# Windowed attention and two feed-forward layers: first chunk's tap products summed and transposed on TensorE, first unit in two halves, another order of softmax, loads and weight preparation

## The reference

```python
w = softmax(weight_gen)                      # over the 7 taps
out = np.einsum('bshk,bskhg->bshg', w, x_unf)  # x_unf: this token and the 6 before
h = x @ w_in1;  g = h * np.cos(h);  x = g @ w_out1
h = x @ w_in2;  g = np.maximum(0.01 * h, h); out = g @ w_out2
```

## Time and profile before

| what | us |
|---|---|
| median of 3 runs | 1177.1 (1176.54 to 1181.43) |
| the profiled execution | 1180.46 |
| its span | 1178.7 |
| PE busy | 1151.8 |
| DVE busy | 905.8 |
| ACT busy | 738.6 |
| POOL busy | 94.8 |

### The profile page before, as it was taken

One profiled execution on the slowest core, in us unless ns is written; L12 is line 12 of the kernel. 1 busy time (PEld: TensorE's weight loads), 2 busy tenths in 40 slices (PEclk: granted clock), 3 DMA queues, 4 the chain that ended last, 5 costly groups with the idle time before them and its releaser, 6 DMA issues.

```text
span 1178.7 us, 23306 instructions
## 1 busy us (share of the span) xinstructions
PE 1151.8 (98%) x10180; PEld 960.2 (81%) x10180; DVE 905.8 (77%) x857; ACT 738.6 (63%) x809; POOL 94.8 (8%) x87
## 2 busy tenths in 40 slices
PE   7879999999999999999999999999999999999998
PEld 5658888887878888888888888888888888888876
DVE  7778798787987869688686978868698786968533
ACT  5657675766847657575665756557575665757544
POOL 4764000000000000000000000000000000000000
PEclk9879999999999999999999999999999999999999
DMA  9400101001010010100001010010101001000000
GB/s 268 144 2 1 34 1 37 12 1 48 1 46 3 1 48 2 48 1 17 32 2 48 2 48 1 1 48 1 48 1 48 2 1 48 1 14 1 9 7 28
DMA packets 15277, 32.68 MB, mean 28 GB/s; under 512 B 5068, under 2 KB 9546, under 8 KB 14920
## 3 DMA queue, kind: packets, MB, share of 16 engines
q1 hardware_dynamic: 15176, 31.19, 8.4%
HBM read 24.89 MB, written 6.29 MB: 26 GB/s over the span
## 4 chain that ended last, share of the span: by engine, by line
PE 90%; DVE 4%; ACT 2%; POOL 2%; issue 1%; ACTq 0%; DVEq 0%; POOLq 0%
PE slot L940 41%; PE acc_a L940 27%; PE acc_b L940 18%; DVE g_lo L710 1%; PE slot L1136 1%; POOL prods L282 1%; DVE gate L774 1%; POOL prods L288 1%; PE acc_b L913 0%; DVE prods L282 0%; PE slot L885 0%; ACT gate L607 0%; ACT L656 0%; ACT whole L603 0%; PE slot L872 0%
## 5 line engine op out<-in xcount | busy, mean ns | idle before, releaser
L940 PE MATMUL acc_a<-g_hi,out_hi_lo 64*128 64x512 f32 x2000 | 698.9, 389 | 0.0
L710 DVE TENSOR_TENSOR g_lo<-gate,g_hi 128x1024 fp32r<-128x1024 f32 x256 | 319.7, 1249 | 115.8 <-ACT g_hi L548 115.2
L940 PEld LDWEIGHTS acc_a<-g_hi,out_hi_lo 64*128 64x128 f32 x2000 | 369.6, 185 | 36.0
L940 PE MATMUL acc_b<-g_hi,out_hi_lo 64*128 64x512 f32 x1000 | 389.8, 390 | 8.9 <-DVE g_lo L710 7.5
L940 PE MATMUL acc_a<-g_lo,out_hi_lo 64*128 64x512 f32 x1000 | 388.1, 388 | 0.0
L940 PE MATMUL acc_b<-g_lo,out_hi_lo 64*128 64x512 f32 x1000 | 387.8, 388 | 0.0
L548 ACT ACTIVATE g_hi<-gate 128x1024 fp32r<-128x1024 f32 x256 | 271.4, 1060 | 104.4 <-PE acc_b L940 82.9
L940 PE MATMUL slot<-x_a_hi,in_a_lo 64*128 64x512 f32 x1024 | 300.8, 395 | 1.6 <-DVE gate L788 1.3
L940 PE MATMUL slot<-x_a_hi,in_a_hi 64*128 64x512 f32 x1024 | 297.2, 388 | 0.0
L940 PE MATMUL slot<-x_a_lo,in_a_hi 64*128 64x512 f32 x1024 | 297.1, 388 | 0.0
L940 PE MATMUL slot<-x_b,in_b_hi 64*128 64x512 f32 x1024 | 296.9, 387 | 0.2 <-DVE x_b L724 0.2
(11 more groups left out here) (87 smaller groups left out, 1058.0 us busy)
## 6 DMA issues: line engine op xcount, KB each, us to landing
x_win<-in_x SPq DMA_DIRECT2D x14, 960.0 KB, 4.7
out<-result SPq DMA_DIRECT2D x16, 384.0 KB, 2.4
out_raw<-in_moe_w_out SPq DMA_DIRECT2D x2, 1024.0 KB, 14.1
taps_w<-in_weight_gen SPq DMA_DIRECT2D x2, 560.0 KB, 8.2
out_raw<-in_moe_w_out SPq DMA_DIRECT2D x2, 512.0 KB, 11.0
in_a_raw<-in_moe_w_in SPq DMA_DIRECT2D x1, 1024.0 KB, 9.0
in_b_raw<-in_moe_w_in SPq DMA_DIRECT2D x2, 512.0 KB, 10.8
in_a_raw<-in_moe_w_in SPq DMA_DIRECT2D x2, 384.0 KB, 6.3
```

The costliest lines, as they stand in the source:

```text
L710: nc.vector.tensor_tensor(g_lo[:, q % 2, :], gate[:, q % 2, :], g_hi[:, q % 2, :].bitcast(FP32), ALU.subtract)\
L940: return nc.tensor.matmul(to, w[rows, :], x[rows, :], start=start, stop=stop)
```

## The change

- **Chunk 0's attention.** DVE only multiplies. Each of the seven products is given to PE, which multiplies it with the identity and accumulates in the slot (`sum_tap`, 16 matmuls of fp32 data for each tap): sum and transposition in one. Four buffers `prods` rotate. `raise_clock` runs 4 products instead of 12, and no more of them between the steps.
- **Softmax.** The first part holds chunk 0 alone, the second chunks 1 and 2; the later parts stand at other steps.
- **First unit.** Its four elementwise stages and the split are done in halves of 512 columns.
- **ACT.** Its queue issues chunk 0's own window; both early Exp stand first; two pieces of columns instead of three stand ahead of `split_high`, and two quarters of `w_out1`'s high part behind it. The third piece follows within steps 0 and 1, with POOL doing its scaling.
- **Loads.** SP loads weights for chunks 0 to 2 first, the column pieces with half of `w_out1` between them, and chunk 1's window last of these.
- **POOL.** Another order, shown below; DVE's last additions of chunk 1 stand one step later (`ATT_END` 6), and the split of chunk 1's input behind the step's pending part.

```diff
-        ATT_DVE, ATT_POOL, ATT_END = 2, 9, 5
+        ATT_DVE, ATT_POOL, ATT_END = 2, 9, 6
-        SOFT_CHUNKS = [(0, 2), (2, 3), (3, 6), (6, 11), (11, C)]
+        SOFT_CHUNKS = [(0, 1), (1, 3), (3, 6), (6, 11), (11, C)]
-        SOFT_START, EXP_AT, SOFT_END = [[(1, 9), (2, 14), (3, 14)], [(1, 13), (2, 16), (3, 16)],
-                                        [(1, 15), (3, 9), (4, 9)]]
+        SOFT_START, EXP_AT, SOFT_END = [[(1, 8), (2, 13), (4, 13)], [(1, 10), (3, 10), (5, 10)],
+                                        [(1, 13), (3, 13), (5, 13)]]
...
-            for instruction in attention(0, dve):
-                instruction()
+            for n in range(taps):
+                if n == 1:
+                    softmax_subtract(1)
+                    dve.wait_ge(x_zeroed, 2 * batch)
+                    dve.wait_ge(halo_loaded[0], 64)
+                if n >= 4:
+                    dve.wait_ge(tap_summed, n - 3)
+                multiply_tap(dve, x_win, 0, taps - 1 - n, n % 4).then_inc(tap_ready, 1)
...
+            def sum_tap(slot, n):
+                tap = prods[:, n % 4, :]
+                def first_dims(j, start=False, stop=False):
+                    for k in range(2):
+                        rows = slice(k * DB, (k + 1) * DB)
+                        ins = nc.tensor.matmul(slot[:, k, j * DB:(j + 1) * DB],
+                                               tap[rows, j * dim:j * dim + DA], ident[rows, rows],
+                                               start=start, stop=stop)
+                    return ins
...
-            raise_clock(12)
-            for n in range(1, ATT_STEPS):
-                pe.wait_ge(att, n)
-                raise_clock(4)
-            pe.wait_ge(att, ATT_STEPS)
-            transpose_input(slots[INPUT_STEP % SLOTS])
+            raise_clock(4)
+            for n in range(taps):
+                pe.wait_ge(tap_ready, n + 1)
+                ins = sum_tap(slots[INPUT_STEP % SLOTS], n)
+                ins.then_inc(tap_summed if n < taps - 1 else filled, 1)
             keep_clock(WARM)
...
-            for n, cols in enumerate(HI_PIECES):
-                act.wait_ge(in_loaded[n], 48)
...
+            act.dma_start(x_win[:, halo:, :].rearrange("p t d -> p (t d)"), x_rows[:, 0:row])\
+                .then_inc(own_loaded[0], 16)
+            exponentials(0)
+            exponentials(1)
+            for n in range(2):
+                column_highs_a(n)
+                column_turns(n)
+                column_highs_b(n)
+            split_high(-1, INPUT_STEP, 0)
+            out_high(0)
+            out_high(1)
+            first_read(-1, STEPS - 1)
+            for step in range(STEPS):
+                step_of(0, step)
+                if step == 0:
+                    column_highs_a(2).then_inc(w1_a_read, 1)
+                if step == 1:
+                    column_highs_b(2)
```

More of the change, by code:

```diff
@@ L313, in attention @@
             yield rest_of_window
[L314 removed]
+            yield third
             yield lambda: tap(3, 3)
@@ L599, in first_read @@
                 slot = slots[step % SLOTS][:, :, :].rearrange("p a n -> p (a n)")
+                if unit(i, q) == 0:
+                    for cols, done in ((slice(0, N), unit_act), (slice(N, None), whole_ready)):
+                        nc.scalar.activation(whole[:, 0, cols], slot[:, cols], ACT.Identity, bias=0.25)\
+                            .then_inc(done, 1)
+                    return
                 if step in FIRST_UNITS:
@@ L624, in step_of @@
                     split_second_high(i, step)
-                if step == FIRST_INPUT_SPLIT and input_splits(i, step):
-                    split_high(i, FIRST_INPUT_STEP, i + 1)
                 if kind(i, step) == "output":
@@ L785, in step_of @@
                     leave_res_b(second_phase(i - 1))
-                if in_first:
+                if in_first and unit(i, q) == 0:
+                    for cols, ready, n, done in ((slice(0, N), unit_act, 2, unit_dve),
+                                                 (slice(N, None), cos_ready, 1, g_ready)):
+                        dve.wait_ge(ready, n)
+                        nc.vector.scalar_tensor_tensor(gate[:, 0, cols], slot[:, cols], RADIANS,
+                                                       gate[:, 0, cols], ALU.mult, ALU.mult)\
+                            .then_inc(done, 1)
+                elif in_first:
                     dve.wait_ge(cos_ready, first_units(i, q))
@@ L879, in transpose_input, with last_dims @@
                 ins.then_inc(filled, 1)
+            def sum_tap(slot, n):
[7 more added lines that the diff above has]
+                    return ins
+                def last_dims(j):
+                    for k in range(2):
+                        rows = slice(k * DB, (k + 1) * DB)
+                        nc.tensor.matmul(slot[0:DB, k, N // 2 + j * DB:N // 2 + (j + 1) * DB],
+                                         tap[rows, j * dim + DA:(j + 1) * dim], ident[rows, rows],
+                                         start=False, stop=False)
+                first_dims(0, start=n == 0)
+                for j in range(J):
+                    last_dims(j)
+                for j in range(1, J):
+                    ins = first_dims(j, stop=n == taps - 1 and j == J - 1)
+                return ins
             def transpose_output(slot):
```

248 lines of the change are left out of this document (172 added, 76 removed).

## The result

The changed kernel is slower by 0.6%: 1185.5 us (median of 4 runs, 1184.57 to 1186.81) against 1177.3 for the kernel before (4 runs, 1176.54 to 1181.43). The ratio is 1.0063, with a 95% interval of 1.0038 to 1.0089, so the loss is small but clear of the noise. The forecast was 1165.6, range 1159 to 1173. The profiled execution took 1184.91, with a span of 1183.1. In what follows the full pace is TensorE's level of 2.4 GHz and the half pace that of 1.2 GHz, told by how long the same instruction takes.

The account below looks back on a forecast made before the run. PE was taken as the bound, fully busy from 350 to 1100 us. Gains of 7.6 at the start (6.6 + 1.0) and 3.9 from the later softmax parts make 11.5: 1177.1 - 11.5 = 1165.6 us, range 1159 to 1173.

Parts of the forecast that it names:

- Step 2: Chunk 0's tap sums on PE: 1.1 us a tap, 2.2 for the first two at half clock, ending at 16.2.
- Tap sums are serial on PE: Rival, chance 0.05: 3.7 us a tap, sums end at 33.5, 17.2 lost, 1182.8 us; slower from 2.9 a tap on.
- Low clock at the first fills: Rival, chance 0.12: fewer products of ones leave three fills and a sum at 1.2 GHz, costing 3.0: 1168.6 us.
- Step 1: Chunk 0's softmax and products on DVE: first product at 6.6 instead of 7.46, the seven products end at 13.4.
- Step 3: The split behind the tap sums: `split_high` at 16.3 instead of 20.55, first fill at 17.7 instead of 21.90; gain 4.2.
- Step 4: First unit in halves: first sum at 28.3 instead of 34.78, gain 6.5; no fall of the clock, 3.0 more.
- Step 5: Chunk 1's input behind POOL's queue: transposes at 56.5 instead of 63.14, gain 6.6; earlier steps' further gain is given back.
- Step 6: Later softmax parts at other steps: 3.9 of PE's 4.19 us idle between 100 and 350 gained; lower bound nothing.

Follow-up runs that it names:

- a7: a1 with only 4 products of ones ahead and none between DVE's steps: 1176.8 us, ratio 0.9996.
- b3: The kernel before with only the first unit in two halves: 1178.6 us, ratio 1.0002.
- b6: The kernel before, unedited, profiled once more: profiled execution 1176.06 us.
- a1: The changed kernel with chunk 0's taps added on DVE as before and the 52 products of ones back: 1175.6 us, ratio 0.9977.
- a2: The changed kernel with 16 instead of 4 products of ones ahead of the tap sums: 1177.3 us, ratio 0.9998.
- a5: The changed kernel with products and identity of the tap sums in fp32r: 1173.8 us, ratio 0.9955.
- a4: a1 with POOL's five products and two additions of chunk 1 replaced by writes of one column each: 1167.1 us, ratio 0.9899.
- b1: The kernel before with only the new steps of the later softmax parts: 1177.5 us, ratio 0.9992.
- c1: a1 with the last quarter of `w_out1`'s lows behind POOL's whole part of chunk 1: 1174.7 us, ratio 0.9969.
- c2: c1 with the third piece of the columns scaled on ACT instead of POOL: 1174.4 us, ratio 0.9978.

## Why the prediction was wrong

**Step 2 failed, and by itself makes the sign.** It took 1.1 a tap at the full level and 2.2 at the half one, for the first two taps only. Measured were 1.65 and 2.95, and all seven taps ran at the half pace. It took twice the lower bound of 0.5 from the transposes' row, and more than three times is what the full level costs; an fp32 product isn't near a transpose of the same shape. With 1.65 the step would have given 8.5 + 7 x 1.65 = 20.0 for the end, 4 behind the forecast 16.2 and level with before. The rest was the clock: the step took the half level for two taps and the full one from then on. In the kernel before, dense products had brought it, 52 of them ahead of the transposes:

```profile
5.88 14.01 PE L1136 MATMUL slot<-g_hi 128*128 128x512 f32 x52 [5.88 <-POOL g_hi L467]
```

In the kernel after PE was busy almost without a gap from 8.48 to the first fill at 32.05, and the pace stayed the half one. So the sums ended at 29.3 instead of 16.2, and from the split to the fill it took 2.63 instead of 1.35 (29.42 to 32.05), as the 12 transposes ran at the half pace as well: 13.1 + 1.3 are the 14.4 by which mark A missed 17.7.

**Two rivals met.** "Tap sums are serial on PE" was priced at 1182.8 with its threshold at 2.9 a tap; 2.95 was measured. "Low clock at the first fills" was 0.12. I gave the first 0.05 because I priced it at the full level; the second is what carries it over its threshold. Both stood apart as small chances, and they are one case. The second had put the half level in the first fills, though, where the kernel after has it only in the first pair of rows; it lay in the sums. That 1182.8 is near the measured 1185.5 is in part luck: this rival had the sums end at 33.5 instead of 29.3, and counted on gains elsewhere that didn't come.

The Trainium skill (FP8 and Floating Point Precision, TensorE Precision Notes) says that true fp32 takes four passes; the estimate from it was 0.9 a tap. Measured at the full level are 1.65. fp32r at the half pace took 1.28 against 2.95 for fp32, a factor of 2.3 for the whole tap, so the passes are not all of its price in products this small.

The Trainium skill (TensorE: Matmul & The Clock Gate, Part 4: PE-mode transpose) says that transposes don't count as work for the gate. The transposes of a7 and of the kernel after run at the half pace (2.82) and don't end it, which agrees; here plain products with an identity, also in fp32r, didn't end it either.

**Step 1** was close: the first product at 7.47 instead of 6.6, since the weights landed at 4.17 instead of near 3.2. The smaller load came later, not sooner. The softmax took 3.30 from there (7.47 - 4.17). The step's own terms (3.2 + 4.06 - 1.44, and at most the 0.62 of the slipped-in reduction) give 5.8 to 6.4, not 6.6.

**Step 3** was right as a mechanism: ACT's pieces were done at 15.95, and `split_high` followed the sums at once, at 29.42. It only had nothing to pass on.

**Step 4** was right in its time for the kernel after: 9.22 from A to B against 10.6 forecast (17.7 to 28.3) and no half level from 34 to 50. But b3 shows that halves alone do nothing, and b6 that the 3.0 for the clock was half of that in an execution near the median: the window's granted clock is 0.76 there, not 0.51.

**Step 5** was right in kind. From the first of the lows (42.90) to the transposes took 29.3 in place of 27.1: the lows of the piece 4.04 instead of 3.3, those of `w_out1` 5.97 instead of 4.4. B to C grew by 3.1 over b6, about what A to B gave (3.5), so that this gain was handed back, as the step had said of all that came before it. It holds for no more than that: the lows begin 1.6 behind B in the kernel after, in a1 and in a7 (42.90, 33.38 and 35.45), and C stands 30.9 behind B in all of them, a2 and a5 too, so an earlier B passes through to C whole. What ate the gain of the new order is that the chain's work grew: from POOL's first product of chunk 1 to C it is 25.3 instead of 19.8 (46.87 to 72.17; 42.78 to 62.55 in b6), with 5.97 of lows of `w_out1` now between the products. a4 shows the most that the chain can give, 8.5.

**Step 6** failed too: 3.9 forecast, and its lower bound, nothing, is what b1 measured. 0.7 of the waits is gone in its profile and two stand in a new place.

The difference in the profiles adds up: against b6, +10.0 at A, -3.5 to B, +3.1 to C, -0.8 to the end, together +8.8 of span; the medians differ by 8.2. With cheaper tap sums the forecast of 11.5 would still not have come: in the medians, each against the kernel before timed with it, a1 gains 2.0, c1 2.7 and a5 3.6. c1 and c2 (1174.7 and 1174.4, 2.7 and 2.6 gained) are the fastest versions with the whole computation in full precision, 0.2 to 0.3% under the kernel before.
